# Moving the first query product, one weight piece and one query load in step 0 of a delta-rule attention kernel

## The chip, the cores and the metric

The kernel runs on one core of one Trainium2 chip. The metric is the device time of one execution in microseconds. TensorE (PE) does matmuls, VectorE (DVE) and ScalarE (ACT) elementwise work and copies, GpSimd (POOL) a few fills, and SyncE (SP) issues the transfers. Weight loads of PE are listed as PEld. Each engine runs its own list of instructions in order and waits on semaphores for the others.

## The reference

Three parts follow one another: an attention with a state that is updated by the delta rule, and two feed-forward networks.

```python
def _attn_ref(q, k, v, beta):                 # (4, 8, 768, 48)
    k_n = k / (norm(k) + 1e-06)
    for t in range(S):
        y[:, :, t] = einsum('bhd,bhde->bhe', q[:, :, t], state)
        v_old = einsum('bhde,bhd->bhe', state, kt)
        state = state + bt * einsum('bhd,bhe->bhde', kt, vt - v_old)

h = x @ w_in;  g = where(h >= 1, h, where(h <= -1, 0, (h + 1) ** 2 / 4));  x = g @ w_out
xn = x / rms * rms_g;  y = (silu(xn @ w_gate) * (xn @ w_val)) @ w_out2
```

## The kernel before, in words

The sequence of 768 tokens is cut into six steps of 128 tokens, each step into two halves of 64. The 32 pairs of batch and head stand side by side, so a step has 64 instances of a 64x64 problem. In a step the attention does this, half by half:

- GK, the product of keys with keys, and its copy to `gram` by ACT (in step 0 one quarter by DVE). DVE turns it into `sysm` ("tr", or in two parts "trh"), takes the norms ("nrm"), scales ("sys"), and inverts blocks of 32 by forward substitution: 31 steps "inv" of two DVE operations each (L975, L979).
- "ft" (L989) and "xd" (L992) turn the inverse into `tt` and `xd`. Z (L1116) and X (L1127) on PE give the block between the two 32-blocks; both use 32x32 matmuls. ACT copies Z (L833) and X (L839). X of half 0 waits for Z's copy and for "xd".
- GQ (L1107) is the product of keys with queries. DVE multiplies it by a mask into `prob` (L1021). "vn" or "vnh" scales v (L998).
- U (L1153) is the inverse times v (less KS, keys times state, L1138, L1030). ACT and in step 0 also DVE copy it to `upd`. KU (L1187) is the update of the state, which DVE adds (L1035). QS (L1160) and PU (L1174) give the attention's output, copied to `v_in`. XT (L1198) turns the output, and "XE" splits it into a high and a low part, `xh` and `xl`, for the first network.

The first network of step k-1 runs on PE between the pieces of step k's attention: h (L1214) and o (L1229), each with three matmuls for high and low parts; ACT and DVE work out g and its parts (L869 to L878, L1046, L1053). The second network (L673, L692) comes last.

Step 0 has no network beside it. In its place stand the weights' low parts: eight chunks of weights are loaded into `stage`, ACT makes the high part of a chunk ("hi", L893), PE sums the difference of weight and high part in PSUM, a third of a chunk at a time ("piece", L1247 and L1248, 24 in all, numbered from 0), and ACT copies it out ("low", L896). A piece uses one of three PSUM banks in turn and waits for the low part of the piece three before. Its matmul on `ident` shows as two records in the trace and the one on `nident` as one, a product of 32 matmuls of an attention unit as 64 records.

The order of all this is a list for each step, `PLANS`. For step 0 it is written by hand in `first_body`; each engine goes through the same list and picks out what is its own. In it the 24 pieces stand between the steps of the inverse, all but the last two. `FIRST` names the PSUM banks of each product of step 0 (0 to 2 are `bank`, 3 and 4 `hps`, 5 to 7 `acc`). A product waits until what was in its banks before has been read: `banks_free` follows the table `BANKS`, worked out from `FIRST` and the order.

U of half 0 waits for v's scaled half (`s_vn`), for ACT's copy of X of half 0 (`s_x`) and for three transposes (`s_ft`). KU waits for U's copies. PU waits for `prob`.

SP issues its transfers in one order. Before the change it waits, behind the loads of step 0, for XT of step 0 (`p_xt`), then issues step 1's queries and the vector `gain`, then goes on to v of step 1, which waits for the same `p_xt`. GQ of step 1 waits for those queries. It stands in the list of step 1 behind the second block of the network's h.

Of the kernel before, what the change touches and what calls it, by code (L numbers as in the profile page):

```python
# [14 lines left out]
KD = DM // P  # L15
# [58 lines left out]
def inversion(c):  # L74

    out = [(("tr", c, n), 20) for n in range(TURNS)] + [(("nrm", c, 0), 14), (("sys", c, 0), 13)]
    out += [(("inv", c, s), 4 + (BLK - 1 - s) * (s + 1) // 48) for s in range(INV)]
    return out + [(("ft", c, 0), 20), (("xd", c, 0), 21)] + [(("ft", c, n), 20) for n in range(1, TURNS)] + [(("vn", c, 0), 17)]
# [15 lines left out]
NPIECE = NCHUNK * PIECES  # L94
# [3 lines left out]
def first_body():  # L98


    out = [("GK", 0, hf) for hf in range(HALVES)]
    pieces = list(range(NPIECE))

    def split(n):

        ev = []
        for p in pieces[:n]:
            ev.append(("piece", 0, p))
            if p >= 2:
                ev.append(("low", 0, p - 2))  # L110
            if p % PIECES == 1 and 2 <= p // PIECES + 1 < NCHUNK:
                ev.append(("hi", 0, p // PIECES + 1))
        del pieces[:n]
        return ev

    for e, _ in inversion(0):
        if e == ("ft", 0, 0):
            break
        if e[0] == "nrm":
            out += [("hi", 0, 0), ("hi", 0, 1)]  # L120
        out.append(e)
        if e[0] == "inv":
            out += split(BESIDE * (e[2] + 1) // INV - BESIDE * e[2] // INV)
            if e[2] == 21:
                out += [("GK", 1, hf) for hf in range(HALVES)]

    def turn(n):

        return [("trh", 1, n)]

    out += split(2) + [("low", 0, NPIECE - 4), ("low", 0, NPIECE - 3)]
    out += [("ft", 0, 0), ("Z", 0, 0), ("Z", 0, 1), ("xd", 0, 0), ("X", 0, 0), ("X", 0, 1), ("ft", 0, 1), ("ft", 0, 2), ("vnh", 0, 0)]
    out += [("GQ", 0, 0), ("piece", 0, NPIECE - 2), ("low", 0, NPIECE - 2), ("U", 0, 0), ("piece", 0, NPIECE - 1)] + turn(0)
    out += [("low", 0, NPIECE - 1), ("KU", 0, 0), ("vnh", 0, 1)]
    out += [("GQ", 0, 1), ("KS", 0, 1), ("GQE", 0, 1), ("PU", 0, 0), ("U", 0, 1), ("QS", 0, 1)] + turn(1)
    out += [("PU", 0, 1)] + turn(2) + turn(3)
    out += [(kind, 0, n) for kind in ("XT", "XE") for n in range(KD)] + [("KU", 0, 1)] + turn(4) + turn(5)
    return out, [e for e in inversion(1) if e[0][0] != "tr"]
# [47 lines left out]
def bodies():  # L186
    plan, left = first_body()
    out = [plan]
    for k in range(1, NSTEP):
# [11 lines left out]

NPSUM = NBANK + 2 + KD
FIRST = {("GK", 0, 0): (0, 1), ("GK", 0, 1): (3, 4), ("GK", 1, 0): (3, 4), ("GK", 1, 1): (0, 1),
# [3 lines left out]

# [77 lines left out]
def build(nc, kq, k, v, beta, w_in, w_out, w_gate, w_val, w_o2, rms_g, y_out, x2d):  # L285
    ctx = ExitStack()
    with ctx:
# [6 lines left out]
        def sem(name):  # L294
            return ctx.enter_context(nc.semaphore(name))
# [25 lines left out]
        with one:  # L321
# [19 lines left out]
            xd = sysm  # L341
# [72 lines left out]
        with psum_one:  # L414
# [13 lines left out]
            p_qs, p_u, p_y, p_ku, p_xt = sem("qs_done"), sem("u_done"), sem("attn_y_done"), sem("ku_done"), sem("xt_done")  # L428
# [35 lines left out]
            def bank_of(u, j=0):  # L464
                return (bank + hps + acc)[BANKS[u][j][0]]
# [35 lines left out]
            def stage_as(n):  # L501
                s = stage[:, n % NSTAGE, :]
                if n < NCHUNK // 2:
                    return s.rearrange("p (k f) -> p k f", k=KD)
                return s.rearrange("p (f n) -> p f n", f=4)
# [190 lines left out]
            with nc.Block() as block:  # L696
                @block.sync
                def _(sp):
                    def load_kq(c, kinds=(0, 1)):
                        if c >= 2:  # L700

                            sp.wait_ge(p_y, HALVES * (c - 1))
                        for a in kinds:
                            for bp in range(BP):
                                sp.dma_start(kqT[c % 2][C * bp:C * bp + D, a, :, :].rearrange("p i t -> p (i t)"), kq[c, a, bp, :, :])\
                                    .then_inc(s_kq[a][c % 2], 16)

                    def load_k(c):
                        if c:

                            sp.wait_ge(p_ku, HALVES * c)
                        sp.dma_start(k_in[:, :, :].rearrange("p i d -> p (i d)"), k[c, :, :]).then_inc(s_k, 16)

                    def load_v(c):
                        if c:

                            sp.wait_ge(p_xt, KD * c)
                        sp.dma_start(v_in[:, :, :].rearrange("p i d -> p (i d)"), v[c, :, :]).then_inc(s_v, 16)

                    def load_w(n):  # L720
                        if n >= NSTAGE:

                            sp.wait_ge(s_wl, PIECES * (n - NSTAGE + 1))
                        sp.dma_start(stage_as(n), w_chunk(w1_src, w2_src, n)).then_inc(s_w[n % NSTAGE], 16)

                    def x2_store(n):
                        for j in range(KD):

                            sp.wait_ge(s_x2, KD * n + j + 1)
                            sp.dma_start(x2d[n, :, j, :], x2s[:, j, :]).then_inc(s_x2d, 16)  # L730

                    for bp in range(BP):
                        sp.dma_start(kqT[0][C * bp:C * bp + D, 0, 0:NPAIR, :].rearrange("p i t -> p (i t)"),
                                     kq[0, 0, bp, :, 0:NPAIR * C]).then_inc(s_k0, 16)
                    for bp in range(BP):
                        sp.dma_start(kqT[0][C * bp:C * bp + D, 0, NPAIR:NINST, :].rearrange("p i t -> p (i t)"),
                                     kq[0, 0, bp, :, NPAIR * C:NINST * C]).then_inc(s_kq[0][0], 16)
                    sp.dma_start(beta_i[:, :, :].rearrange("p c t -> p (c t)"), beta[:, :]).then_inc(s_beta, 16)

                    sp.wait_ge(s_kq[0][0], 16 * BP)  # L740
                    for n in range(NSTAGE):
                        load_w(n)
                    load_kq(1, (0,))
                    load_w(NSTAGE)
                    load_v(0)
                    load_w(NSTAGE + 1)
                    load_kq(0, (1,))
                    for n in range(NSTAGE + 2, NCHUNK):
                        load_w(n)
                    load_k(0)  # L750

                    sp.wait_ge(p_xt, KD)
                    load_kq(1, (1,))
                    sp.dma_start(gain[:, :], rms_g.rearrange("(k p) -> p k", p=P), allow_slow_non_contiguous=True).then_inc(e_gain, 16)

                    def after(n, f):

                        sp.wait_ge(s_h, NF1 * n + f + 1)

                    for c in range(1, NSTEP):  # L760

                        load_v(c)
                        if c + 1 < NSTEP:
                            after(c - 1, 0)
                            load_kq(c + 1, (0,))
                        after(c - 1, 2)
                        load_k(c)
                        if c > 1:
                            x2_store(c - 2)
                        if c + 1 < NSTEP:  # L770
                            after(c - 1, 4)
                            load_kq(c + 1, (1,))

                    sp.wait_ge(p_y, HALVES * (NSTEP - 1))
                    for n in range(2):
                        load_x2(sp, n)

                    sp.wait_ge(s_xl, NSTEP * KD)
                    load_w2(sp, 0)
                    load_w2(sp, 1)  # L780
                    x2_store(NSTEP - 2)
                    for r in range(2, len(W2_ORDER)):
                        load_w2(sp, r)
                    x2_store(NSTEP - 1)
                    second_sync(sp)
# [129 lines left out]
                def _(dve):  # L915
                    def attention(u):
                        kind, c, q = u
# [16 lines left out]
                        elif kind == "trh":  # L934
                            q, s0 = divmod(q, 2)
# [76 lines left out]
                        elif (kind, c, q) == ("PU", 0, 1):  # L1012
                            dve.wait_ge(p_y, half(c, q))
                            dve.tensor_copy(v_in[:, NINST - H:NINST, :].rearrange("p i d -> p (i d)"),
                                            bank_of(out_of(c, q), 1)[:, 0:BIG]).then_inc(s_y2, 1)
                        elif (kind, c, q) == ("GQE", 0, 1) or kind == "GQ" and (c, q) != (0, 1):
                            hf, u = q, ("GQ", c, q)
                            dve.wait_ge(p_gq, half(c, hf))
                            for j in range(NQH):
# [272 lines left out]
```

## Time and profile before

| | |
|---|---|
| median of 3 runs | 1081.17 us (1079.69 to 1082.04) |
| profiled execution, its own time | 1083.05 us |
| its span | 1081.2 us |
| PE busy | 1044.9 us (97%) |
| DVE busy | 578.8 us (54%) |
| ACT busy | 418.7 us (39%) |
| mean granted clock of PE | 0.988 |

The span runs from the first to the last instruction of the profiled execution; all places below are in us from its start. PE is busy almost throughout, but a busy PE is not PE at full speed: a matmul counts as busy for its duration, and that doubles where the granted clock is 0.50. The inverse of step 0 runs on DVE up to 42.6 us, Z and X follow, and the first matmul of the first network stands at 76.06 us. So the region that the change touches lies between 30 and 90 us, while the span is over ten times as long; what happens there must be read from views cut to that region.

### The profile page before, as it was taken

The page shows a single profiled execution, that of the slowest core. Times are in us where ns is not written, and L with a number is a line of the kernel's source. Part 1 is how long each engine was busy: PE and PEld are TensorE (multiplying, and loading weights), DVE is VectorE, ACT ScalarE, POOL GpSimd, SP SyncE. Part 2 cuts the span into 40 slices and gives each one's busy share as a digit, 9 for nine tenths or more (in the row PEclk, how much of TensorE's full clock was granted, in tenths as well). Part 3 has the DMA queues.
Part 4 walks back from the last instruction along what each step waited for, and adds up shares of the span by engine and source line. Part 5 has one row for each costly group of instructions (what it writes and reads, how often), then busy time and mean ns, then how long its engine had stood idle before and what let it go on. Part 6 is the DMA issues. An engine that isn't in the chain of part 4 may idle for free.

```text
span 1081.2 us, 24182 instructions
## 1 busy us (share of the span) xinstructions
PE 1044.9 (97%) x10828; PEld 849.3 (79%) x10828; DVE 578.8 (54%) x983; ACT 418.7 (39%) x673; POOL 9.6 (1%) x20
## 2 busy tenths in 40 slices
PE   6888999999999999999999999999999999999996
PEld 4566677777777777777778888888888888888885
DVE  5869768858948857873356535323324334333322
ACT  5622444454354454444476643232132232232211
POOL 1000000000000000000000000000000000000000
PEclk9888999999999999999999999999999999999999
DMA  8424002300500320030030230200200200100101
GB/s 248 137 35 114 2 3 60 89 2 31 118 3 3 71 78 3 31 118 2 3 117 29 88 116 2 55 4 1 59 1 1 59 1 1 30 1 1 30 1 29
DMA packets 19031, 48.05 MB, mean 44 GB/s; under 512 B 2448, under 2 KB 9232, under 8 KB 17872
## 3 DMA queue, kind: packets, MB, share of 16 engines
q1 hardware_dynamic: 18928, 46.51, 15.8%
q8 instruction: 85, 1.39, 0.5%
q14 instruction: 18, 0.15, 0.0%
HBM read 37.06 MB, written 9.44 MB: 43 GB/s over the span
## 4 chain that ended last, share of the span: by engine, by line
PE 83%; DVE 13%; issue 3%; ACT 1%; POOL 0%; DVEq 0%; POOLq 0%; ACTq 0%
PE bank L673 21%; PE acc L1229 15%; PE hps L1214 15%; PE acc L692 10%; PE hps L673 7%; PE hps L692 4%; DVE inv L979 3%; DVE outer L975 3%; PE bank L1127 1%; PE bank L1153 1%; DVE g L1046 1%; DVE g1l L1053 1%; PE bank L1116 1%; DVE prob L1021 1%; PE bank L1160 1%
## 5 line engine op out<-in xcount | busy, mean ns | idle before, releaser
L590 ACT ACTIVATE g<-bank 128x512 f32<-128x512 f32 x72 | 43.1, 598 | 257.3 <-PE bank L673 142.6
L1214 PE MATMUL hps<-xh,w1h 128*128 128x512 f32 x288 | 121.8, 423 | 5.1 <-DVE g L1046 5.0
L1229 PE MATMUL acc<-g1h,w2h 128*128 128x512 f32 x288 | 120.2, 417 | 1.7 <-DVE g1l L1053 1.6
L878 ACT ACTIVATE g1h<-g 128x512 fp32r<-128x512 f32 x96 | 60.7, 632 | 157.8 <-DVE g L1046 145.1
L1214 PE MATMUL hps<-xh,w1l 128*128 128x512 f32 x288 | 115.0, 399 | 0.0
L1214 PE MATMUL hps<-xl,w1h 128*128 128x512 f32 x288 | 114.9, 399 | 0.0
L1229 PE MATMUL acc<-g1l,w2h 128*128 128x512 f32 x288 | 114.3, 397 | 0.0
L1229 PE MATMUL acc<-g1h,w2l 128*128 128x512 f32 x288 | 114.0, 396 | 0.0
L1053 DVE TENSOR_TENSOR g1l<-g,g1h 128x512 fp32r<-128x512 f32 x96 | 66.2, 690 | 69.1 <-ACT g1h L878 68.6
L1046 DVE SCALAR_TENSOR_TENSOR g<-hps,g 128x512 f32<-128x512 f32 x96 | 65.7, 685 | 61.6 <-ACT g L872 61.3
L869 ACT ACTIVATE g<-hps,half_c 128x512 f32<-128x512 f32 x96 | 65.6, 683 | 58.3 <-PE hps L1214 58.3
L632 DVE TENSOR_TENSOR pr<-g,hps 128x512 f32<-128x512 f32 x36 | 24.7, 687 | 111.0 <-ACT g L590 111.0
L632 DVE TENSOR_TENSOR pr<-g,bank 128x512 f32<-128x512 f32 x36 | 24.7, 686 | 111.1 <-ACT g L590 111.1
L635 DVE TENSOR_TENSOR g1l<-pr,g1h 128x512 fp32r<-128x512 f32 x72 | 49.8, 692 | 51.1 <-ACT g1h L599 51.1
L599 ACT ACTIVATE g1h<-pr 128x512 fp32r<-128x512 f32 x72 | 45.5, 632 | 71.7 <-DVE pr L632 70.1
L692 PE MATMUL acc<-w2h,g1l 128*128 128x384 f32 x216 | 72.6, 336 | 0.0
L692 PE MATMUL acc<-w2h,g1h 128*128 128x384 f32 x216 | 72.6, 336 | 0.0
L692 PE MATMUL acc<-w2l,g1h 128*128 128x384 f32 x216 | 72.5, 336 | 0.0
L1214 PEld LDWEIGHTS hps<-xh,w1h 128*128 128x128 f32 x288 | 54.6, 189 | 22.0 <-DVE g L1046 9.6
L1229 PEld LDWEIGHTS acc<-g1h,w2h 128*128 128x128 f32 x288 | 54.4, 189 | 17.7 <-DVE g1l L1053 4.1
L979 DVE TENSOR_TENSOR inv<-inv,outer 128x31 f32<-128x31 f32 (+15 forms) x186 | 63.9, 343 | 6.4
L1214 PEld LDWEIGHTS hps<-xh,w1l 128*128 128x128 f32 x288 | 54.8, 190 | 13.3
(196 smaller groups left out, 2033.2 us busy)
## 6 DMA issues: line engine op xcount, KB each, us to landing
kqT<-kq SPq DMA_DIRECT2D x22, 384.0 KB, 6.4
v_in<-v SPq DMA_DIRECT2D x6, 768.0 KB, 4.3
k_in<-k SPq DMA_DIRECT2D x6, 768.0 KB, 5.6
x2d<-x2s SPq DMA_DIRECT2D x18, 256.0 KB, 5.6
x2t<-x2d SPq DMA_DIRECT2D x6, 768.0 KB, 5.6
y<-y_t SPq DMA_DIRECT2D x48, 96.0 KB, 2.2
stage<-w_in SPq DMA_DIRECT2D x4, 768.0 KB, 8.0
stage<-w_out SPq DMA_DIRECT2D x4, 768.0 KB, 10.0
```

The costliest lines, as they stand in the source:

```text
L599: act.activation(prh[:, f % 2, :], pr[:, f % 2, :], ACT.Copy).then_inc(e_prh, 1)
L632: dve.tensor_tensor(pr[:, f % 2, :], silu[:, f % 2, :], vps[f % 2][:, :], ALU.mult).then_inc(e_pr, 1)
L635: dve.tensor_tensor(prl[:, f % 2, :], pr[:, f % 2, :], prh[:, f % 2, :].bitcast(F32), ALU.subtract).then_inc(e_prl, 1)
L673: last = pe.matmul(ps[:, :], wt[:, kk, P * f:P * f + P], xx[n % 2][:, kk, :], start=(e == 0), stop=(e == 3 * KD - 1))
L692: last = pe.matmul(yps[j][:, 0:DM], pp[:, f % 2, js], wt[:, f, :], start=(f == 0 and e == 0), stop=(f == NF2 - 1 and e == 2))
L869: act.activation(g1[:, f % 2, :], hps[f % 2][:, :], ACT.Relu, bias=half_c[:, 0:1], scale=0.5)\
L878: act.activation(g1h[:, f % 2, :], g1[:, f % 2, :], ACT.Copy).then_inc(s_gh, 1)
L979: dve.tensor_tensor(inv[:, s + 1:BLK, 0:w], inv[:, s + 1:BLK, 0:w], tmp, ALU.subtract).then_inc(s_inv, 1)
L1046: dve.scalar_tensor_tensor(out=g1[:, f % 2, :], in0=hps[f % 2][:, :], scalar=1.0, in1=g1[:, f % 2, :], op0=ALU.max, op1=ALU.min).then_inc( ...
L1053: dve.tensor_tensor(g1l[:, f % 2, :], g1[:, f % 2, :], g1h[:, f % 2, :].bitcast(F32), ALU.subtract).then_inc(s_gl, 1)
L1214: last = pe.matmul(hps[f % 2][:, :], wt[:, kk, P * f:P * f + P], xx[:, kk, :], start=(kk == 0 and e == 0), stop=(kk == KD - 1 and e == 2))
L1229: last = pe.matmul(acc[j][:, :], wt[:, f, P * j:P * j + P], gg[:, f % 2, :], start=(f == 0 and e == 0), stop=(f == NF1 - 1 and e == 2))
```

## The change

GQ of step 0, half 0, is done by PE after piece 16 and step 26 of the inverse, instead of after X. DVE's multiplication of it stays where it was, behind the scaling of v, under the name "GQE", as half 1 had it already; so GQ keeps its two PSUM banks from then on. For this its banks become 2 and 0, and Z of half 0 and X of half 1 both use bank 1. Piece 22 moves from behind GQ to a place between Z and X; ACT's copy of it keeps its place. SP issues step 1's queries and `gain` without waiting for XT.

```diff
@@ first_body
+            if e[2] == 26:
+                out.append(("GQ", 0, 0))
...
-    out += [("ft", 0, 0), ("Z", 0, 0), ("Z", 0, 1), ("xd", 0, 0), ("X", 0, 0), ("X", 0, 1), ("ft", 0, 1), ("ft", 0, 2), ("vnh", 0, 0)]
-    out += [("GQ", 0, 0), ("piece", 0, NPIECE - 2), ("low", 0, NPIECE - 2), ("U", 0, 0), ("piece", 0, NPIECE - 1)] + turn(0)
+    out += [("ft", 0, 0), ("Z", 0, 0), ("Z", 0, 1), ("piece", 0, NPIECE - 2), ("xd", 0, 0), ("X", 0, 0), ("X", 0, 1), ("ft", 0, 1), ("ft", 0, 2), ("vnh", 0, 0)]
+    out += [("low", 0, NPIECE - 2), ("GQE", 0, 0), ("U", 0, 0), ("piece", 0, NPIECE - 1)] + turn(0)
@@ FIRST
-         ("Z", 0, 0): (0,), ("Z", 0, 1): (3,), ("X", 0, 0): (4,), ("X", 0, 1): (2,), ("GQ", 0, 0): (1, 0), ("U", 0, 0): (3, 4),
+         ("Z", 0, 0): (1,), ("Z", 0, 1): (3,), ("X", 0, 0): (4,), ("X", 0, 1): (1,), ("GQ", 0, 0): (2, 0), ("U", 0, 0): (3, 4),
@@ SP
                     load_k(0)
-
-                    sp.wait_ge(p_xt, KD)
                     load_kq(1, (1,))
@@ DVE
-                        elif (kind, c, q) == ("GQE", 0, 1) or kind == "GQ" and (c, q) != (0, 1):
+                        elif kind == ("GQ" if c else "GQE"):
```

## Rows read from the trace of the kernel before

**Rows 1.** The page's chain that ended last, shares by engine
```profile
PE 83%; DVE 13%; issue 3%; ACT 1%; POOL 0%; DVEq 0%; POOLq 0%; ACTq 0%
```

**Rows 2.** PE's waits, 80 to 120 us: total us, times, longest us
```profile
PE hps L1214 <- DVE g L1046: 4.6, 3, 2.1
PE bank L1107 <- DMA kqT<-kq: 2.9, 1, 2.9
```

**Rows 3.** Busy time by stretch: length, PE, PEld, DVE, ACT, POOL, clock, DMA, GB/s
```profile
80.00:90.00 10.00, 5.17 (x75) 3.95 (x74) 9.35 (x29) 3.14 (x6) 0.00 (x0) 0.78 0.81 161
...
130.00:600.00 470.00, 468.11 (x6888) 366.82 (x6887) 313.04 (x564) 227.72 (x390) 2.86 (x3) 1.00 0.16 44
```

**Rows 4.** The chain that ended last, step 0: start us, us, what
```profile
47.09 1.71 issue
...
52.00 2.06 PE bank L1107 x64
54.06 2.00 PE acc L1247 x2
...
56.49 1.89 PE hps L1153 x64
...
59.67 0.91 PE bank L1187 x64
...
62.09 0.97 issue
...
65.74 0.84 issue
66.58 1.08 PE bank L1153 x59
...
69.09 1.42 issue
```

**Rows 5.** PE's timeline: start us, us, instruction, count, idle before and its releaser
```profile
30.73 1.16 PE L1097 MATMUL hps<-kqT 48*64 48x64 f32 x64
...
32.75 1.12 PE L1247 MATMUL acc<-stage,ident 128*128 128x512 f32 x2
...
38.46 1.02 PE L1247 MATMUL acc<-stage,ident 128*128 128x512 f32 x2
...
44.72 1.17 PE L1116 MATMUL bank<-tt,gram 32*32 32x32 f32 x63 [0.54 <-DVE tt L989]
```

**Rows 6.** Busy time by stretch, around the changes of the granted clock
```profile
44.60:48.01 3.41, 2.38 (x144) 2.32 (x145) 3.41 (x2) 1.41 (x3) 0.00 (x0) 1.00 0.02 5
...
54.84:58.26 3.42, 3.42 (x67) 2.14 (x65) 0.58 (x1) 0.60 (x1) 0.00 (x0) 0.50 0.00 0
61.67:65.08 3.41, 2.34 (x128) 2.17 (x128) 1.68 (x3) 0.00 (x0) 0.00 (x0) 1.00 0.02 5
```

**Rows 7.** Busy time by stretch, from gap to gap
```profile
48.75:62.50 13.75, 13.00 (x379) 10.04 (x379) 6.92 (x9) 4.03 (x7) 0.95 (x1) 0.65 0.01 4
62.50:66.20 3.70, 2.35 (x126) 2.16 (x126) 1.98 (x4) 0.87 (x2) 0.00 (x0) 1.00 0.02 4
```

**Rows 8.** Tile kqT, transfers issued from 22 to 25 us
```profile
DMA to landing us min/median/max: 9.8/11.1/12.3
```

**Rows 9.** Tile stage, 29 to 30 us: the issue of chunk 7, its landing
```profile
L724 SPq DMA_DIRECT2D stage<-w_out x1: 384/384/384, 29.2 to 29.2; - x1
...
DMA to landing us min/median/max: 10.3/10.3/10.3
```

**Rows 10.** SP's timeline
```profile
75.24 0.80 SPq L705 DMA_DIRECT2D kqT<-kq  x2
```

**Rows 11.** Timelines of DVE (first row) and ACT (second row)
```profile
50.03 0.96 DVE L998 TENSOR_TENSOR v_in<-v_in,ntok 128x768 f32<-128x768 f32 x1
...
52.04 1.19 ACT L839 ACTIVATE tt<-bank 32x512 f32<-32x512 f32 x2 [0.52 <-PE bank L1127]
```

**Rows 12.** DMA queues, 36 to 37 us: packets, MB, share of 16 engines
```profile
q8 instruction: 1, 0.02, 6.9%
```

## Prediction

> **What bounds the kernel now.** I began with the page's chain of work that ended last [rows 1]: 83% of it is PE and 13% DVE, so time is saved only where one of them stands on it. Then the list of PE's waits from 80 to 120 us [rows 2], since the change moves a load that is wanted there: PE waits once 2.9 us for a kqT transfer and three times, 4.6 us together, for DVE.
>
> The busy time by stretch [rows 3] says what a saving is worth. From 80 to 90 DVE is busy 9.35 of 10 us, and goes on so until about 113: step 1's inverse, small operations each waiting for the one before. From 130 to 600 PE is busy 468.11 of 470. So what makes step 0 end earlier starts DVE's work earlier and moves everything behind it by as much. What only frees PE between 80 and 113 gives nothing, since behind the kqT wait PE goes on to wait for DVE's g.
>
> The chain through step 0 [rows 4]: PE does Z (from 44.72 [rows 5]), begins X, stands 1.71 us, ends X at 52.00, then GQ of half 0 (2.06), weight piece 22 (2.00, and 0.43 to 56.49), U (1.89), piece 23 (1.29 to 59.67), KU. GQ and piece 22 need nothing of X; they merely stand ahead of U on PE. Their durations are double those elsewhere: the granted clock, 1.00 (2.4 GHz) while PE did Z, was 0.50 (1.2 GHz) behind the gap, still from 54.84 to 58.26 while PE did piece 22 and U without a pause, and 1.00 again when KU was done [rows 6].
>
> **The gap of 1.71 us.** X had begun when PE stopped, so its semaphores had been given: it is no wait for data. Three more gaps for "issue" follow, 0.97, 0.84 and 1.42 [rows 4]. Between the first two stand 379 matmuls, between the next 126, each with a weight load [rows 7]: 3 and 1 times about 256 instructions. I read the gaps as loading of code in blocks of 256 instructions, begun when the block before is entered. The block ahead of a gap is entered 128 matmuls earlier: about 45.0, 59.7, then 63.06 and 66.58. The next is usable at 48.80, 63.06, 66.58 and 70.51, so 3.8, 3.4, 3.5 and 3.9 us after. PE stalls where it eats a block faster. The Trainium skill's page "Runtime: NRT & Kernel Launch" (Instruction fetch mechanics) gives PE room for 2048 instructions and calls the crossing of a block mostly hidden; the trace does not agree, with its gaps of 0.84 to 1.71 us. By that rule the first gap would have another cause and stay, and X would end about 1 us later than in the sum below.
>
> **The change, part by part.** Times are of the profiled execution (span 1081.2, own time 1083.05, which is 1.9 above the median of 1081.17); I carry the difference over to the median.
>
> *GQ among the pieces.* It follows piece 16, at 38.46 [rows 5]. Its queries, issued between 22 and 25, land at most 12.3 us after issue [rows 8], by 37.3 at the latest, so it doesn't wait. The two GK products of the same shape took from 30.73 to 32.75 [rows 5], so one costs 1.01 at full clock. PE does the pieces back to back and then idles 0.54 before Z; so Z moves by +0.5, to 45.2. ACT's copies have slack for that. Behind X, 2.06 us go.
>
> *Banks.* Z half 0 and X half 1 now share bank 1. The latter needs ACT's copy of the former, done by about 47.2, and comes at 49.5: nothing. GQ keeps banks 2 and 0 until DVE multiplies it, which it does behind v's scaling, as now; KU and GQ of half 1 want them later: nothing.
>
> *Piece 22 between Z and X.* 144 matmuls of Z and X took 2.38 us [rows 6], so Z's 128 take 2.1, to 47.3. The piece then lasts 1.1 (piece 23 took 1.29, partly slow), to 48.4; X would run to 50.6. With 64 more matmuls ahead of Z, a block is now entered in the new GQ, and the next with the 17th matmul of Z half 1, at 46.5. It runs out at the 13th of X half 1, at 49.7, and the next is usable at 46.5 + 3.4 to 3.9 = 49.9 to 50.4. The gap shrinks from 1.71 to between 0.2 and 0.7; the piece, six instructions in over a microsecond, is what gives it the time. The rest of X takes 0.85: it ends at about 51.0.
>
> *U.* It also waits for v's scaling, done at 50.03 + 0.96 = 50.99 [rows 11], and for ACT's copy of X half 0 (two copies, 1.19 [rows 11], from 49.6: 50.8). All three meet: U starts at 51.1 instead of 56.49. DVE's order is unchanged, and its multiplies of GQ fit beside U.
>
> *U to KU.* At full clock U takes 1.08 (as in half 1 [rows 4]) and the piece 1.29: 53.5, and ACT, with two copies of X, the low part of piece 22 and U's copy, is ready at about 53.6. Gain 59.67 - 53.6 = 6.1. At 1.2 GHz U takes 1.89 and the piece 2.43: KU at 55.4, gain 4.3.
>
> Which clock? What PE did before it fell was Z, in 32x32 matmuls, and idling. From 61.67 to 65.08 it was busy no more (2.34 against 2.38 us), with 48x64 matmuls, and it didn't fall [rows 6]. The new stretch from 45.2 to 51.1 is still Z and X, with one full piece in it. I take it that the clock falls once, between X and the end of U, and returns by the end of piece 23, as it did behind piece 22 and U. Fallen early in X it costs more (gain 3.6), late in U less (5.2). I take 4.5.
>
> *Behind KU.* As many instructions stand ahead of it as before, so blocks fall as before: the gaps of 0.97, 0.84 and 1.42 stay.
>
> *Step 1's queries and the gain vector.* Two transfers of 384 KB and a small one are issued behind k_in, at about 30, instead of from 75.24 [rows 10], and SP, with nothing else to issue, spends about 1.2 us on them. Then it waits for XT, as before, for v. PE's wait of 2.9 us goes and becomes a longer wait for g: worth 0, the cover being DVE's chain; 2.9 if that cover were gone. The bytes now share the DMA engines with the last loads. They are queued behind weight chunk 7, issued at 29.2 and landed 10.3 later [rows 9], at 39.5; its first reader comes at about 41.3: 1.8 of slack. k_in is wanted only by KU. So the price is 0, or, were all 0.79 MB put ahead of chunk 7 at the 161 GB/s of 80 to 90 us [rows 3], 4.9 - 1.8 = 3.1. I take 0, by the order of issue.
>
> Sum: -4.5 (Z's +0.5 is in it), 0, 0. Median 1081.17 - 4.5 = 1076.7; the span, 1081.2 - 4.5, is 1076.7 too.
>
> **The rivals.**
> *Full clock throughout.* If piece 22 keeps the clock up, 6.1 come off: 1075.1. For it, the gaps left are short; against, Z and X are still most of the stretch. Chance 0.25.
> *The 2.9 us were real.* If PE, not DVE, set the pace at 80 us, 4.5 + 2.9 come off: 1073.8. Against: DVE is full there. 0.05.
> *Contention.* The block entered in GQ, at 39.0, is fetched beside the moved queries. By the count, a block was entered at about 31.4, in GK, with the DMA engines loaded; its 0.02 MB of instructions show only from 36 to 37 [rows 12]. If the new fetch waits for the last query, about 45.5, Z stalls 1.5 us; chunk 7 late costs up to 3.1. So 1.4 to 3.0 are left, say 2.5: 1078.7. The Trainium skill's page "DMA: Bandwidth & Descriptors" (Queues, rings and completion order) has each DMA engine take turns between queues packet by packet, by which the fetch would hardly wait; the trace shows some 4.6 us. 0.12.
> *The clock stays down.* The low spell ended behind GQ, piece 22 and U; two of these no longer stand there. If the clock doesn't return before XT, U (0.8), the piece (1.1) and the seven products behind them (0.9 each) cost 8.2 more, of which the three gaps (3.2) absorb all or nothing: 5.0 to 8.2. It decides from 6.1: 1080.1 to 1083.3. Against: from 54.84 the piece and U alone brought it back. 0.08, half of it slower.
>
> **The numbers.** The forecast has 0.50 and its own range is 3.6 to 5.2 off, 1076.0 to 1077.6. The range of 1074.0 to 1079.3 takes in full clock and most of contention, and about 1 us for the spread of the runs shown (1079.69 to 1082.04). A measurement here tells 0.2%, 2.2 us, from no change. Faster 0.88, same 0.08, slower 0.04.
>
> **What would show it.** GQ near 38.5, Z near 45.2; no gap over 1 us in X; U near 51.1; KU at 55.4 (53.6 if the clock is 1.00 there); the same gaps in KS, U and PU; no wait for kqT, a longer one for g. I am wrong if a gap opens in Z, if U waits for something else, or if the clock is 0.50 past KU.

## The result and the profile after

The changed kernel takes 1077.52 us in the median (1075.42 to 1079.37, 9 runs), the kernel before 1081.17 (1078.87 to 1082.04, 9 runs). The ratio is 0.9967, 95% interval 0.9958 to 0.9977: faster by 3.6 us, between 2.5 and 4.5. The profiled execution took 1077.52 us, its span is 1075.7. That is 5.5 less than the span before, while the medians differ by only 3.6; the other 1.9 is taken up below.

First the chain of the changed kernel's page, to set beside [rows 1], and PE's waits from 80 to 120 us, beside [rows 2]:

```profile
PE 82%; DVE 14%; issue 3%; ACT 1%; POOL 0%; DVEq 0%; POOLq 0%; ACTq 0%
```

```profile
PE hps L1214 <- DVE g L1046: 7.7, 5, 4.3
PE acc L1229 <- DVE g1l L1053: 0.5, 1, 0.5
```

The kqT row is gone and the g row has grown, from 4.6 to 7.7: 3.1, where the transfer had held 2.9. The load bought nothing but another wait. The chain that ended last, beside [rows 4]:

```profile
51.36 1.15 PE hps L1153 x64
52.51 1.06 PE acc L1247 x2
53.80 0.91 PE bank L1187 x64
...
56.21 1.37 issue
...
60.39 0.71 issue
61.10 1.84 PE bank L1153 x59
64.91 0.41 PE hps L1174 x2
67.14 0.57 DVE v_in L1014
67.84 1.94 PE bank L1198 x8
```

U stands at 51.36 instead of 56.49 and KU at 53.80 instead of 59.67. The gap in X has gone, and no GQ or piece 22 stands between X and U. PE's timeline, beside [rows 5], shows GQ among the pieces, Z 0.4 later than before, and what U waited for:

```profile
38.36 1.16 PE L1107 MATMUL bank<-kqT 48*64 48x64 f32 x64
...
45.12 0.57 PE L1116 MATMUL bank<-tt,gram 32*32 32x32 f32 x24
...
51.36 1.15 PE L1153 MATMUL hps<-v_in,tt 64*64 64x48 f32 x64 [0.38 <-DVE v_in L998]
```

The busy time by stretch, beside [rows 6] (length, PE, PEld, DVE, ACT, POOL, clock, DMA share, GB/s), shows the clock: 1.00 through X, U and KU, and 0.50 in the tail of step 0, for 13.65 us:

```profile
48.50:51.00 2.50, 2.44 (x129) 2.18 (x128) 2.47 (x2) 1.18 (x2) 0.72 (x1) 1.00 0.00 0
51.36:59.00 7.64, 5.98 (x297) 4.91 (x299) 4.67 (x8) 2.41 (x5) 0.00 (x0) 1.00 0.02 4
59.08:72.73 13.65, 12.02 (x306) 11.02 (x298) 8.60 (x14) 3.64 (x7) 0.00 (x0) 0.50 0.07 16
80.00:90.00 10.00, 7.78 (x84) 6.16 (x85) 9.55 (x25) 3.79 (x6) 0.00 (x0) 0.68 0.21 76
```

The gaps that are left can be set beside the DMA queue for instructions. In this trace its transfers of 16 KB start at 55.16, 58.72 and 62.14 us; the first two have landed at 56.24 and 59.67, and PE resumes 1.3 and 1.4 us later, at 57.58 and 61.10. From 55.1 to 56.3 us:

```profile
q8 instruction: 1, 0.02, 5.7%
```

In the two profiles, the lead of the changed kernel goes so: 5.9 us at KU (59.67 against 53.80), 5.5 at KS past its gap (63.06, 57.58), 4.6 at XT (72.41, 67.84), 4.3 at the last transposes for step 1's inverse (77.52, 73.22) and all through that inverse, then 5.5 from the tenth g of step 1 (134.83, 129.30) to the end. The step back is the low clock in the tail; the step up is the kernel before, whose clock fell at 116.28 where the changed one's did not. Neither belongs to the change as such: in a second profile of the changed kernel (span 1075.8) the clock stayed up in the tail until 66.42, step 1's inverse began 5.65 ahead (76.93 against 82.58), and the clock fell at 110.79.

### The profile page after: what moved, and what is told of

It is laid out like the page before. It is cut to its first block, busy times and chain, and to the rows that moved or that the text cites. A ratio compares the mean times of both kernels' runs of the same rounds, so it can differ in the third digit from the quotient of the medians.

```text
span 1075.7 us, 24182 instructions
## 1 busy us (share of the span) xinstructions
PE 1043.0 (97%) x10828; PEld 848.3 (79%) x10828; DVE 579.0 (54%) x983; ACT 418.6 (39%) x673; POOL 9.6 (1%) x20
## 4 chain that ended last, share of the span: by engine, by line
PE 82%; DVE 14%; issue 3%; ACT 1%; POOL 0%; DVEq 0%; POOLq 0%; ACTq 0%
PE bank L675 21%; PE hps L1214 15%; PE acc L1229 15%; PE acc L694 10%; PE hps L675 7%; PE hps L694 4%; DVE inv L979 3%; DVE outer L975 3%; DVE g L1046 1%; PE bank L1153 1%; DVE tt L989 1%; PE bank L1127 1%; DVE prob L1021 1%; PE bank L1187 1%; PE bank L1174 1%
## 5 line engine op out<-in xcount | busy, mean ns | idle before, releaser
L637 DVE TENSOR_TENSOR g1l<-pr,g1h 128x512 fp32r<-128x512 f32 x72 | 49.8, 692 | 51.1 <-ACT g1h L601 51.1
L975 DVE TENSOR_TENSOR outer<-sysm,inv 128x31 f32<-128x31 f32 (+15 forms) x186 | 62.9, 338 | 3.7
```

The lines of the kernel that those rows point to most:

```text
L637: dve.tensor_tensor(prl[:, f % 2, :], pr[:, f % 2, :], prh[:, f % 2, :].bitcast(F32), ALU.subtract).then_inc(e_prl, 1)
L975: dve.tensor_tensor(tmp, sysm[:, s, s + 1:BLK].unsqueeze(2).to_broadcast([P, n, w]), inv[:, s:s + 1, 0:w].to_broadcast([P, n, w]), ALU.mul ...
```

## The experiments

All ratios are to the kernel before, timed beside each version; its median moved between 1080.51 and 1081.76 us from one group of versions to the next.

**The query product alone.** Of the changed kernel, piece 22 and the wait on SP are put back:

```diff
-    out += [... ("Z", 0, 1), ("piece", 0, NPIECE - 2), ("xd", 0, 0), ...
-    out += [("low", 0, NPIECE - 2), ("GQE", 0, 0), ...
+    out += [... ("Z", 0, 1), ("xd", 0, 0), ...
+    out += [("piece", 0, NPIECE - 2), ("low", 0, NPIECE - 2), ("GQE", 0, 0), ...
+                    sp.wait_ge(p_xt, KD)
                     load_kq(1, (1,))
```

> Only GQ of step 0, half 0, moves among the pieces (with its banks and the later multiplication); piece 22 stays between X and U, and step 1's queries wait for XT. By the theory of work in the way and of code blocks of 256 instructions: Z at 45.15 as in the changed kernel; X begins at 47.4 instead of 48.5, eats its block by the 16th matmul of half 1, at 48.7, and stands there 1.1 to 1.6 us, since that block was entered at 46.4; X ends near 51.1, piece 22 near 52.3 (53.6 at half clock), KU begins between 55.0 and 57.5 (before 59.67, changed kernel 53.80). Time 2.2 to 4.5 us under the kernel before. Rival, that the gap in X is a fixed cost of X (a hand-over or a wait for data): a gap of 1.7 us stays at the 16th matmul of X half 0.

Measured: 1077.56 us, 0.9967 (0.9954 to 0.9980). This edit alone gives what the whole change gives. The chain (line numbers are two higher here):

```profile
48.34 0.24 PE bank L1129 x15
48.57 0.99 issue
49.56 0.95 PE bank L1129 x49
50.51 1.06 PE acc L1249 x2
51.57 0.23 PE acc L1250
51.80 1.08 PE hps L1155 x64
```

The gap is not in X of half 0 but at the 16th matmul of half 1 (15 run, 49 remain), as the count of blocks had it, so it belongs to no product. It is 0.99 instead of 1.1 to 1.6, and the clock stays up, so KU comes at 54.16, earlier than forecast and only 0.4 behind the changed kernel. Piece 22 between X and U costs little, because without it U would wait for DVE's v, done at 51.20, anyway.

**The piece alone.** The same on the kernel before: piece 22 between Z and X, GQ behind X.

> Only piece 22 moves between Z and X; GQ stays behind X, and step 1's queries wait for XT. Theory: Z at 44.72; the gap in X shrinks from 1.71 to 0.2 to 0.7 at about the 13th matmul of X half 0 (at 48.2), X ends at 50.5; a new gap of 1.3 to 1.8 opens in GQ near its 13th matmul at full clock (none at half clock, where GQ is slower than the loading); KU at 55.7 at full clock, 57.4 at half. Time 2.3 to 4.0 us under the kernel before. So the two parts alone would bring together more than both at once, because each gives the code loading the same time. Rival, that the parts are plain sums of durations (GQ 2.06, piece 2.43): this one brings 2.4 and the other 2.1 at KU, with the gap of 1.71 in place.

Measured: 1079.78 us, 0.9983 (0.9974 to 0.9991).

```profile
48.63 0.98 PE hps L1127 x50
...
50.65 0.38 PE bank L1107 x12
51.03 1.12 issue
52.14 0.97 PE bank L1107 x50
...
53.17 1.60 PE hps L1153 x61
```

In X 0.05 us is left; the new gap opens in GQ after 12 matmuls, 1.12 long. KU is at 56.97. Beside a kernel before at 1081.76 us, GQ alone gives 4.2, the piece alone 2.0 and both together (the version without the query load, below) 4.1 us. The parts overlap, as the theory of blocks had it, though the intervals of the ratios are too wide to show that by themselves. The profiles show it better: KU comes 5.5 and 2.7 us earlier with one part, 5.9 with both. The rival of plain sums fails by the gap in X, which it wanted in place.

**The query load alone, and everything but it.** The wait on SP taken from the kernel before, and put back into the changed one:

> The kernel before, with only the wait for XT ahead of step 1's queries and the gain vector taken away (they are loaded behind k_in). Theory (DVE's inverse covers PE's wait): PE's wait for kqT of 2.9 us is gone, its wait for DVE's g at the same place grows by as much, the first multiplication of g and all of DVE's steps of the inverse stand where they did, and the time is within 0.1% of the kernel before. Rival, that the 2.9 us were on the path: 1078.3, or 0.27% faster. Third, contention with the last weight chunks: step 0 later by up to 3 us.

> The changed kernel with the wait for XT put back ahead of step 1's queries. Theory: KU at 53.8 and the same time as the changed kernel within 0.1% (about 0.33% under the kernel before); PE waits some 3 us for kqT again, hidden. Rival: 0.27% slower than the changed kernel.

Measured: 1081.60 us, 0.9995 (0.9986 to 1.0003), and 1077.63 us, 0.9967 (0.9956 to 0.9978). Worth nothing either way: the interval of the first leaves at most 1.5 us. PE's waits in it from 80 to 120:

```profile
PE hps L1212 <- DVE g L1044: 8.2, 4, 4.6
PE acc L1227 <- DVE g1l L1051: 0.5, 1, 0.5
```

The profiled execution of the second was a late one (1082.79 us against its median of 1077.63), and shows where executions differ. ACT's waits from 28 to 45 us, and PE's:

```profile
ACT w2h L895 <- DMA stage<-w_out: 6.4, 3, 4.6
```

```profile
PE acc L1249 <- ACT w2l L898: 3.7, 1, 3.7
```

Weight chunk 5 landed 3.1 us late (at 35.04 instead of 31.93; ACT waited 4.6 for it against 2.7 in the changed kernel's profile). PE stood 3.7 us ahead of piece 15. The clock fell in that wait, at 38.16, and was back at 44.99, so that pieces 15 and 16 and GQ ran at half clock and the last five pieces at full. Z began at 51.06 instead of 45.12. This happened with the moved load not there, so it isn't its doing.

**Half a block more ahead.** In the changed kernel GK of step 1, half 0, is done twice:

```diff
-                            for h in range(H):
+                            for h in [h for _ in range(2 if (c, hf) == (1, 0) else 1) for h in range(H)]:
```

> The changed kernel with GK of step 1, half 0, done twice into the same banks at 31 us (64 matmul records, 128 instructions more ahead of everything that follows; PE idles 1.9 us behind it, which covers its 1.0 us). If the gaps are loading of code in blocks of 256 instructions, all of them move 64 matmul records earlier: none in KS, U of half 1 or PU of half 1; instead 1.2 to 1.7 us near the 9th matmul of U of half 0, and gaps near the 5th of GQ half 1, the 3rd of PU half 0 and the 2nd of QS half 1. KU then starts 1.0 to 1.5 us later than in the changed kernel, but the end of PU half 1 moves by less than 0.5, as the number of blocks up to there is nearly the same. If the gaps are waits of those products for data or hand-overs, they stay in KS, U and PU, and nothing moves.

Measured: 1083.53 us, 1.0014 (1.0002 to 1.0026): 5 us slower than the changed kernel, which I had not expected.

```profile
33.36 0.69 PE bank L1097 x46
34.05 5.61 issue
39.66 0.90 PE bank L1097 x18
...
61.90 0.72 issue
...
64.67 0.16 PE acc L1174 x4
64.83 1.38 issue
...
67.35 0.88 PE bank L1153 x60
68.29 1.54 issue
69.83 0.25 PE hps L1160
```

The gaps of the tail are where half a block earlier puts them: in GQ, behind the 4th matmul of PU half 0, and at the start of QS. None is left in KS or U. The one in U of half 0 did not come: ACT's copies of X held U until 58.45, past the arrival. But the shift also brings a boundary into GK itself, which eats 128 matmuls in 2 us while the weight chunks load, and there PE stands 5.61 us. In the kernel before, the fetch of that block began about as late (36.12, here 37.17), but it was wanted only at 45. So the theory of blocks held, and its price under load was missing from my sum.

**The last piece late.** Piece 23 and its low part go between GQ and KS of half 1.

```diff
-    out += [("low", 0, NPIECE - 2), ("GQE", 0, 0), ("U", 0, 0), ("piece", 0, NPIECE - 1)] + turn(0)
-    out += [("low", 0, NPIECE - 1), ("KU", 0, 0), ("vnh", 0, 1)]
-    out += [("GQ", 0, 1), ("KS", 0, 1), ...
+    out += [("low", 0, NPIECE - 2), ("GQE", 0, 0), ("U", 0, 0)] + turn(0)
+    out += [("KU", 0, 0), ("vnh", 0, 1)]
+    out += [("GQ", 0, 1), ("piece", 0, NPIECE - 1), ("low", 0, NPIECE - 1), ("KS", 0, 1), ...
```

> The changed kernel with piece 23 (and ACT's copy of it) moved from between U and KU of half 0 to between GQ and KS of half 1, where PE stands 1.37 us in the changed kernel. Theory of blocks: KU begins as soon as U is copied, at 53.3 instead of 53.80, but KS resumes only about 3.7 us behind the 6th matmul of KU, at 57.1 to 57.6, so the piece is free there and little is won by the order itself (0 to 0.4 us). If full-size matmuls in that place keep the granted clock at 1.00 through U, QS, PU of half 1 and XT (in the changed kernel it was 0.50 from 59.08 to 72.7), another 1.0 (PU), 0.9 (XT) and 0.6 (KU of half 1) come off: 2.5 us. If not, the time equals the changed kernel's within 0.1%.

Measured: 1078.14 us, 0.9963 (0.9951 to 0.9975), the changed kernel's time within the noise. KU begins at 53.71, no earlier: U's copies (ACT's ends at 53.46) had been hidden by the piece. The clock was 1.00 throughout:

```profile
51.00:80.00 29.00, 18.62 (x687) 15.40 (x681) 20.98 (x42) 7.85 (x16) 0.23 (x1) 1.00 0.25 58
```

Step 1's inverse began 1.1 us earlier than in the changed kernel, and 1.2 were lost again at 110.6, where the clock fell.

**The second product cut.** 28 of GQ's 32 matmuls of half 1 are left out, so its time is that of a kernel with less work:

```diff
-                            for h in range(H):
+                            for h in range(H - 1 if (c, hf) == (0, 1) else 0, H):
```

> The changed kernel with GQ of step 0, half 1, cut to its last head (4 of 32 matmuls; the rest of the product is left out, so the output is not the reference's): 112 instructions fewer between KU and KS. If the tail of step 0 is bound by the loading of code blocks, one every 3.5 to 3.9 us whatever PE does, this is worth far more than its 0.9 us: the gap of 1.37 in KS goes, the next ones come 56 matmul records later (in PU half 0, QS half 1 and XT), and PU of half 1 ends 2 to 3 us earlier than in the changed kernel (67.08). If the gaps are data waits, it is worth at most 0.9 us at KS and the gap in KS only grows.

Measured: 1077.66 us, 0.9961 (0.9950 to 0.9973): nothing beyond the changed kernel. The gaps come 56 matmul records later (behind the 61st of KS and the 59th of U, not where I had named them), so the last block still ends inside PU by the count:

```profile
58.14 0.41 issue
...
60.13 1.10 PE bank L1153 x59
61.23 1.40 issue
62.62 0.32 PE bank L1153 x5
```

From KU to PU of half 1 it is 9.7 us (54.83 to 64.51), in the changed kernel's second profile 9.4 (53.73 to 63.16). Some 0.6 of the 9.7 is the clock, which fell here at 63.22. So 0.9 us less of matmuls buys about 0.3: the tail pays by the block while as many blocks are entered. My 2 to 3 us were wrong; the count behind them was careless.

**Fillers.** Full-size matmuls on constants that nobody reads, in PE's waits: eight in the tail of step 0, six ahead of h of block 7 in step 1.

```diff
+                            for _ in range({("KS", 0, 1): 3, ("U", 0, 1): 2, ("XT", 0, 0): 3}.get(u, 0)):
+                                pe.matmul(bank_of(u)[:, :], nident[:, :], w1h[:, 0, 0:512], start=True, stop=True)
...
+                            if (kk, n, f) == (0, 0, 7):
+                                pe.wait_ge(s_gq, quarter(1, 0, 1))
+                                for _ in range(6):
+                                    pe.matmul(bank[1][:, :], nident[:, :], w1h[:, 0, 0:512], start=True, stop=True)
```

> The changed kernel with full-size matmuls on constants, not read by anyone, where PE waits in the tail of step 0: 3 ahead of KS half 1, 2 ahead of U half 1, 3 ahead of XT (0.23 us each at full clock). Theory: they stand in gaps and cost nothing; KS still resumes 3.7 us behind the 6th matmul of KU (a block isn't there sooner because PE asks later); what they may bring is the clock: if it stays at 1.00 where it was 0.50 from 59.08 to 72.7, PU half 1, XT and KU half 1 take 2.6 us less and step 1's inverse begins 1 to 2 us earlier than at 78.28, as in the kernel with the late piece (77.16, clock 1.00). Median up to 0.1% under the changed kernel. Rival (a block is there 2.3 us after entry, and PE only pays more when it comes too early): KS runs through without a gap and PU ends 1 us earlier even at equal clock.

> The changed kernel with six such unread full-size matmuls (1.4 us) ahead of h of block 7 in step 1, where PE waits 2.12 us for DVE's g, the last such wait before PE is full. Theory: that wait sometimes drops the clock for the 3.4 us behind it (before, query load only, piece only, late piece: 1.2 us lost between the end of step 1's inverse and the tenth g; changed kernel and two others: not lost). With the fillers it is never lost: the tenth g comes 20.9 us behind the last step of the inverse in every profile, and the median is 0.3 to 0.8 us under the changed kernel, with a smaller spread. Rival: the clock falls all the same, or the fillers delay h: equal or slower by up to 1.4.

> The changed kernel again, beside the three others on one chip, as their reference and for a second profile. Theory: 0.3 to 0.4% under the kernel before; KU at 53.8; the same blocks; the clock's low spells at other places than in the first profile.

Measured: 1077.88 us, 0.9968 (0.9957 to 0.9980); 1077.06, 0.9963 (0.9952 to 0.9974); the changed kernel again 1077.57, 0.9963 (0.9951 to 0.9975). With the tail's fillers the clock was 1.00 up to 80.8, and KS resumed 4.0 us behind KU's 6th matmul although PE asked for the block only 2.9 us behind its predecessor's entry, instead of 2.4:

```profile
57.74 0.24 PE hps L1140 x2
57.98 1.03 issue
59.01 0.20 PE acc L1140
```

That settles it between "a block comes 2.3 us behind entry, and being early is punished" and "it is usable 3.1 to 4.1 behind, whatever PE does": the second. By the first, PE would not have had to wait here. With the fillers of step 1 the clock kept 1.00 through the wait:

```profile
108.00:122.00 14.00, 12.43 (x145) 9.36 (x146) 12.97 (x18) 4.17 (x7) 0.83 (x1) 1.00 0.01 2
```

and the tenth g came 20.97 us behind the last step of the inverse. Without fillers it is 22.1 where the clock falls there, in 8 of 11 profiles (the kernel before and the changed kernel's second among them), and 20.9 in the other 3, the changed kernel's first among them. With these fillers it didn't fall in any of 3 profiles. In the medians none of it can be told from the changed kernel.

**Both together.** The late piece with step 1's fillers, and all fillers:

> The changed kernel with both edits that kept the clock up where it costs: piece 23 late (between GQ and KS of half 1) and six unread full-size matmuls ahead of h of block 7 in step 1. Theory: no low spell between U of half 0 and the first h (late piece: step 1's inverse begins 23.4 us behind KU, against 24.55 in the changed kernel's first profile), and the tenth g 20.9 us behind the end of step 1's inverse. Together 0.5 to 2 us under the changed kernel: median 1075.5 to 1077. Rival: the low spells only move, and the median is the changed kernel's (0.9965 of before).

> The changed kernel with the unread matmuls of both earlier filler kernels (8 in the tail of step 0, 6 in step 1). Theory: clock at 1.00 from Z to the long wait at about 80 us and again through the waits at 105 to 115; the tail's eight cost 0.3 us where they delay a block's entry. Median 0 to 1 us under the changed kernel, and a spread of runs below its 4 us. Rival: no difference in either.

Measured: 1076.87 us, 0.9968 (0.9958 to 0.9978), and 1077.10, 0.9975 (0.9963 to 0.9987). Their profiles have the shortest spans, 1074.8 and 1074.5, with no low spell but the harmless one near 80. From 104 to 130 us of the first:

```profile
104.00:130.00 26.00, 24.43 (x396) 18.69 (x395) 18.53 (x25) 12.11 (x21) 0.95 (x1) 1.00 0.01 2
```

But the medians don't follow, and the spread did not shrink (1075.86 to 1079.87, and 1075.48 to 1082.11). Where it comes from is not shown. In two profiles above their kernel's median (1082.79 us without the query load, 1079.79 with step 1's fillers) ACT waited 4.6 and 4.5 us for weight chunk 5. No version here beats the changed kernel by more than can be told.

## Why the prediction was right, and where it was not

*What bounds the kernel.* Right. The lead at the inverse of step 1 was kept through it to a tenth of a microsecond, and PE was full from 130 on (468.09 of 470 us).

*The gap as loading of code.* Shown: moving half a block moved the gaps by half a block, cutting 56 records moved them by 56, and in the profiles of the kernel before and of the changed one PE resumes 1.3 to 1.6 us after a transfer on the instruction queue has landed. The Trainium skill's page "Runtime: NRT & Kernel Launch" (Instruction fetch mechanics), with room for 2048 instructions and crossings that are mostly hidden, doesn't describe these gaps of 0.3 to 1.7 us. I forecast 0.2 to 0.7 in X and 0 was left (0.32 in the second profile).

*GQ among the pieces, banks, piece 22, U.* Right in the places: Z at 45.12 for 45.2, X's end at 50.98 for 51.0, U at 51.36 for 51.1, with DVE's v as the last to come. The piece's own share was overrated: with GQ alone the time is the same.

*Which clock.* This is the step that failed: "I take it that the clock falls once, between X and the end of U". In none of the 11 profiles with GQ among the pieces did it fall between X and KU; in all three with GQ behind X it did (48.01, 47.1, 53.2). KU came at 53.80, the figure of the rival "full clock throughout" (53.6), a lead of 5.9. Why the clock stayed up is not shown: in the kernel with GQ alone a gap of 0.99 stood in X and it didn't fall, in the one with the query load alone a gap of 0.96 and it did.

*The total was right through a second error.* The 5.9 did not reach the median, for two reasons. The clock fell later instead, in the tail: U, QS and PU of half 1 took 5.98 us (61.10 to 67.08) instead of 5.07 (66.58 to 71.65), although the gap of 1.42 in PU was gone. By XT 1.3 us of the lead were given back, by step 1's inverse 1.6. That was one of the prediction's signs of being wrong ("if the clock is 0.50 past KU"). In the second profile only 0.3 were given back there, but the lead did not grow again behind step 1's inverse, since the clock fell in both kernels. And "I carry the difference over to the median" was unsound: the profiled execution before was 1.9 above its median, and part of its bad luck lay in the very place that was costed. The query load alone, in which step 0 has the same order, shows a gap of 0.96 in X instead of 1.71 and KU at 58.8. Against that profile the changed kernel's KU leads by 5.0 and its span is 4.1 shorter. The spans of the two costed profiles, before and changed, differ by 5.5; less the 1.9, that is the 3.6 of the medians. That the forecast of 4.5 lies near the measured 3.6 is therefore in part luck: two errors cancel. How the rest splits between blocks of code that arrive 0.4 to 0.5 later and the clock is within the scatter of single profiles, and stays open.

*Behind KU.* "The same gaps" held in place, not in size: 1.37, 0.71 and none for 0.97, 0.84 and 1.42. At half clock PE took 4.0 us for a block (61.10 to 65.13), as long as the next took to come, so the last gap closed. In the second profile, at full clock there, it was 1.42 again.

*The load.* Worth 0 in three kernels; the cover was DVE's inverse, and the rival of 2.9 us is refuted. ACT didn't wait for chunk 7. The fetch of the block entered in GQ did start late: entered at 38.88 by the count, fetched from 43.00. Slack hid it in the changed kernel, but with the moved load there a gap opened in Z in two of nine profiles, of 0.35 us with the late piece and of 0.68 with the tail's fillers. So this rival was half right in its mechanism and cost nothing that the medians show. The Trainium skill's turns between queues ("DMA: Bandwidth & Descriptors", Queues, rings and completion order) would make fetches nearly immune to load; the 5.61 us in GK speaks against that. That the other transfers are what delays a fetch is argued from the two falling together. Where GQ was entered behind their end (the late profile without the query load: last landing 44.12, entry about 44.6), the fetch began at 45.04; with GQ alone moved they had landed at 41.44 and the fetch, due since 38.35 by the count, began at 42.57.

## What to carry to other kernels

Work that needs nothing of the serial chain can be taken from between two links and put where another engine sets the pace, even at a small delay there; look for it right ahead of the product that everything waits for. It pays only up to the next thing that this product waits for: with GQ gone, piece 22 hid nothing but a wait for DVE's v, and moving it too brought nothing more. A wait in the list is worth something only if the next instruction of that engine isn't held by another: read the following row too. And compare a costed stretch over more than one profile before its size is trusted, since a profile at the slow end of the spread has its excess somewhere, perhaps in just that stretch.

## What the runs showed of the hardware

- The streams of small matmuls here are bound by their instructions: 128 matmul records with their weight loads (256 instructions) run in about 2.1 us, but the next such block is usable only 3.1 to 4.1 us after one is entered (3.05 with the query load alone, 4.08 with the second product cut), whatever PE does between.
- With the DMA engines full that time grew to 7.7 us: entered at 32.0 by the count, usable at 39.66 (GK done twice).
- The granted clock fell in or behind short gaps (1.71 and 0.96 us in X, 1.12 in GQ), but not behind one of 0.99 in X. Behind the wait for g near 110 us (2.1 us) it fell in 8 of 11 profiles, and in none of 3 when full-size matmuls filled 1.3 us of it. The same program had low spells at different places in each execution: from 59.08 for 13.65 us in one profile of the changed kernel, and for 3.4 us at 66.4 in the other.
